# Weight splits and small set-up steps moved in the opening of a fused delta-rule attention, MLP and routed-expert kernel

## What is computed

```python
# 1: delta-rule attention, for each of the 32 batch*head pairs
k_n = k / (norm(k) + 1e-06)
for t in range(S):
    y[t] = q[t] @ state
    state += beta[t] * outer(k_n[t], v[t] - k_n[t] @ state)
# 2: MLP on the 3072 tokens (384 -> 2048 -> 384)
h = x @ w_in
x = maximum(0.01 * h, h) @ w_out
# 3: skip test, then the best of 8 experts (384 -> 1024 -> 384) for each token kept
do_compute = x @ w_skip > 0
e = argmax(xc @ w_gate); out = xc + gate_w * (relu(xc @ w1[e]) @ w2[e])
```

## Time and profile before

| | us |
|---|---|
| median of 3 runs | 889.0 |
| lowest and highest of the three | 887.79 and 889.74 |
| the profiled execution | 887.79 |
| its span, first to last instruction | 886.0 |

### The profile page before, as it was taken

One profiled execution on the slowest core, in us unless ns is written; L12 is line 12 of the kernel. 1 busy time (PEld: TensorE's weight loads), 2 busy tenths in 40 slices (PEclk: granted clock), 3 DMA queues, 4 the chain that ended last, 5 costly groups with the idle time before them and its releaser, 6 DMA issues.

```text
span 886.0 us, 27697 instructions
## 1 busy us (share of the span) xinstructions
PE 776.4 (88%) x10782; PEld 624.0 (70%) x10783; DVE 661.4 (75%) x1333; ACT 496.1 (56%) x1108; POOL 416.3 (47%) x498
## 2 busy tenths in 40 slices
PE   0134689999999999999999999999999899999985
PEld 0134567777878787777787788878777677778764
DVE  6758978888888888888888787866868773553382
ACT  4543566667676767666666666555465552442261
POOL 5212254545362636354554535352353665565473
PEclk9995799999999999999999999999999999999998
DMA  9869666676777697767677676336515864363100
GB/s 214 222 115 209 130 103 115 131 132 128 131 133 147 135 138 148 128 129 135 129 130 123 129 138 123 77 66 208 180 29 205 273 231 157 104 197 113 40 17 17
DMA packets 357245, 119.76 MB, mean 135 GB/s; under 512 B 330418, under 2 KB 348388, under 8 KB 356752
## 3 DMA queue, kind: packets, MB, share of 16 engines
q1 hardware_dynamic: 351424, 104.33, 56.6%
q0 software_dynamic: 3200, 7.64, 2.6%
q10 hardware_dynamic: 2512, 6.29, 2.1%
HBM read 63.53 MB, written 21.25 MB: 96 GB/s over the span
## 4 chain that ended last, share of the span: by engine, by line
PE 35%; DVE 23%; issue 11%; ACT 9%; DMA 9%; SPq 7%; POOL 5%; DVEq 0%; POOLq 0%; ACTq 0%
PE b_acc L848 8%; PE b_h L742 7%; PE b_acc L755 7%; PE b_h L835 6%; DVE stage L1484 4%; PE b_ch L681 4%; SPq L497 3%; DVE inv L1410 3%; DVE inv L1416 3%; DMA t_dram<-inv 3%; ACT ga L953 2%; ACT operands L953 2%; DMA operands<-t_dram 2%; ACT stage L1073 1%; PE b_gr L643 1%
## 5 line engine op out<-in xcount | busy, mean ns | idle before, releaser
L1908 POOL TENSOR_TENSOR stage<-stage 128x256 f16<-128x256 f32 x192 | 143.1, 746 | 251.2 <-ACT stage L953 250.3
L742 PE MATMUL b_h<-stage,wt 128*128 128x256 f16 x1728 | 222.3, 275 | 7.9 <-DVE stage L1343 5.4
L755 PE MATMUL b_acc<-wt,stage 128*128 128x384 f16 x1152 | 219.3, 327 | 2.5 <-POOL stage L1908 1.6
L742 PEld LDWEIGHTS b_h<-stage,wt 128*128 128x128 f16 x1728 | 159.1, 98 | 28.7 <-DVE stage L1343 7.5
L755 PEld LDWEIGHTS b_acc<-wt,stage 128*128 128x128 f16 x1152 | 107.0, 98 | 57.6 <-POOL stage L1908 4.5
L953 ACT ACTIVATE stage<-stage 128x256 f16<-128x256 f32 x192 | 80.0, 417 | 106.5 <-DVE stage L1484 105.5
L1484 DVE SCALAR_TENSOR_TENSOR stage<-b_h,stage 128x256 f32<-128x256 f32 x192 | 80.7, 420 | 42.1 <-ACT stage L1073 40.6
L848 PE MATMUL b_acc<-wt,operands 128*128 128x384 f16 x552 | 98.8, 330 | 7.3 <-DVE operands L1524 7.3
L835 PEld LDWEIGHTS b_h<-y,wt 128*128 128x128 f16 x1656 | 93.5, 98 | 6.5 <-issue 4.6
L835 PE MATMUL b_h<-y,wt 128*128 128x128 f16 x1656 | 96.5, 220 | 1.5 <-DVE y L1343 0.7
L1416 DVE TENSOR_REDUCE inv<-inv 128x30 f32<-128x90 f32 (+4 forms) x180 | 85.0, 472 | 5.8
(11 more groups left out here) (215 smaller groups left out, 1289.0 us busy)
## 6 DMA issues: line engine op xcount, KB each, us to landing
operands<-in_moe_w_dram SPq DMA_DIRECT2D x18, 1536.0 KB, 7.3
a_sys<-a_dram SPq DMA_DIRECT2D x24, 256.0 KB, 4.4
kc<-operands SPq DMA_DIRECT2D x22, 256.0 KB, 4.3
natq<-in_q_dram SPq DMA_DIRECT2D x24, 192.0 KB, 4.0
raw_v<-in_v_dram SPq DMA_DIRECT2D x24, 192.0 KB, 4.1
stage<-y SPq DMA_DIRECT2D x96, 48.0 KB, 2.0
x_dram<-stage SPq DMA_DIRECT2D x24, 192.0 KB, 2.9
out_dram<-stage SPq DMA_DIRECT2D x24, 192.0 KB, 3.4
```

The lines of the kernel that those rows point to most:

```text
L742: mm = pe.matmul(b_h[f % 2][:, 0:GT], wt[0][:, a, d * FF + f * P:d * FF + (f + 1) * P], xT[:, g % 2, b, d, :], start=(i == 0), stop=(i == ...
L755: mm = pe.matmul(b_acc[w][:, 0:DM], g16[:, f % 4, a, w * P:(w + 1) * P], wt[1][:, b, f * DM:(f + 1) * DM], start=(f == 0 and (a, b) == PAR ...
L1908: pool.tensor_tensor(g16[:, f % 4, LO, :], g32[:, f % 4, :], g16[:, f % 4, HI, :], ALU.subtract).then_inc(g_lo, 1)
```

## The change

Six things are moved or exchanged; the arithmetic is the same.

1. `split_w_in(2)` goes behind the start of W_out's load on ACT, and behind `norm(2)` on DVE.
2. `a21_high(0)` goes ahead of `q_high(0)` on ACT, and `a21_low(0)` from behind `inverse_low(0)` to a place ahead of `q_low(0)` and of the inverse on DVE.
3. `split_w_out(0)` and `(1)` on ACT go from ahead of `inverse_high(0)` to behind the last `p_high(0)`, with `seed(1)` between them. On DVE they stay where they were.
4. The zeroing of `kn[2]` goes from POOL to DVE.
5. In its place POOL issues a plain DMA of 128 single values (`row_id`, ready by then) to a new scratch tensor in DRAM that nobody reads. Its completion adds 16 to `yo_scattered`.
6. The waits on `yo_scattered` count 16 more, and tile 0, which had none, has one as well.

```diff
@@ ScalarE
             for st in range(B):
                 gram_out(0, st)
-            split_w_in(2)
+            a21_high(0)
             for x in range(2):
                 q_high(0, x)
             act.wait_ge(const_pool, 1)
             seed(0)
-            a21_high(0)
             act.wait_ge(a_loaded[0], 32)
             load_w_out(0)
+            split_w_in(2)
             squares(2)
             first_z()
-            for i in range(2):
-                split_w_out(i)
             inverse_high(0)
...
             for st in range(2, B):
                 p_high(0, st)
+            split_w_out(0)
             seed(1)
+            split_w_out(1)
             act.wait_ge(t_loaded, 128)
             load_w_out(1)
@@ VectorE
             kn_low(1)
             split_w_in(1)
-            split_w_in(2)
+            zeros(kn[2])
+            a21_low(0)
             for x in range(2):
                 q_low(0, x)
             inverse(0, 0, LINKS)
             inverse_low(0)
-            a21_low(0)
             for r in range(2):
                 scan_z_low(0, r)
             norm_sum(2)
             norm(2)
+            split_w_in(2)
@@ GpSimd
-            pool.memset(kn[2].bitcast(F32), 0.0).then_inc(zeroed, 1)
+            pool.dma_start(spare_dram, row_id[:]).then_inc(yo_scattered, 16)
...
-                if not (isinstance(t, int) and t == 0):
-                    pool.wait_ge(yo_scattered, 16 * t)
+                pool.wait_ge(yo_scattered, 16 * t + 16)
                 pool.sem_inc(yo_left, 1)
...
-            pool.wait_ge(yo_scattered, 16 * total)
+            pool.wait_ge(yo_scattered, 16 * total + 16)
```

More of the change, by code:

```diff
@@ L72, in build @@
         t_dram = nc.dram_tensor("t_dram", (2, 4, NU, 2, HR, BLK), F16, kind="Internal").ap()
+        spare_dram = nc.dram_tensor("spare_dram", (P, 1), F32, kind="Internal").ap()
         ident = sb("ident", [P, P])
```

## The result

| | before | changed |
|---|---|---|
| median of 7 runs each, us | 887.79 | 895.81 |
| lowest and highest, us | 886.92, 889.74 | 891.07, 896.93 |
| the profiled execution, us | 887.79 | 895.62 |
| its span, us | 886.0 | 893.9 |
| the same, to the start of the first W_in matmul | 98.06 | 105.50 |

The changed kernel takes 1.0075 times as long, 95% interval 1.0052 to 1.0097 (an estimate from all runs of both kernels; the two medians alone would give 1.0090). The forecast was 889.8, the range 887.2 to 892.2: the time lies above both. Of 7.9 us more of span, 7.44 are there when the first W_in matmul starts (98.06 before, 105.50 now), and the rest of the program took 788.4 against 787.9. So the loss is in the opening, as everything in the argument was. All lines of the changed kernel are one higher than before, POOL's behind the new DMA two.

What follows compares the result with a forecast made beforehand. DVE's in-order list up to the first W_in matmul was taken as the bound, SP's chain second. Terms +0.6 (with -1.37 in it), 0, 0, 0.2 and 0 gave +0.8 us: forecast 889.8, range 887.2 to 892.2.

Steps and rivals of the forecast that it cites:

- the small DMA's price: POOL's new DMA just before a_sys is read: delays a_sys by 0.2 us, bounds 0 and 0.92.
- Rival C: The extra DMA holds up a_sys, so the inverse starts after 37; 2.6 us in place of 0.2, 892.2 us; chance 0.12.
- What bounds the kernel: Opening up to the first W_in matmul: DVE's in-order list bounds, SP's chain 0.92 us behind; shifts carry unchanged to the end.
- Ahead of the inverse: DVE before the block inverse: 0.84 us more work fits in idle time; the inverse still starts when a_sys lands, cost 0.
- a21_low: Leaves the chain between inverse and norm_sum, so root, gram_out(1) and masked tiles come 1.37 us earlier; bounds 0 and 1.37.
- Rival D: The 1.37 us isn't gained, as POOL at nat_k(2) or PE's gram tiles end as late; 891.1 us; chance 0.11.
- split_w_in(2) behind norm(2): DVE's 2.29 us piece fits in 3.03 us of idleness, slowing nat_k(2) on POOL to 3.29; cost 0, other end 0.7.
- The two W_out copies: On ACT between last p_high and u's high half: +1.95 us before any gain, net +0.6 with the 1.37 counted in.
- Tile loop: One fused register step per tile in POOL's sequencer, 97 ns at most, 20 times; taken as 0, far end 0.6.

Runs made afterwards that it cites:

- h1: The changed kernel with the small DMA's 128 values of 4 bytes each written to a row of 512 bytes of its own; 889.70 us, ratio 1.0022.
- f2: The changed kernel with the same 128 values sent from ACT's queue, ahead of a21_high(0), instead of POOL's; 898.19 us, ratio 1.0112.
- h2: The changed kernel with only 8 of the small DMA's 128 values written, side by side; 891.08 us, ratio 1.0031.

## Why the prediction was wrong, step by step

**The failed step is the small DMA's price.** The sum had it at 0.2 us, from the cost of a packet on q1 and q0, bounds 0 and 0.92. It measured 6.67 at the inverse. The DMA's packets did cost next to nothing: the trace has 32 of them, two for each of 16 engines and not 8, and they were gone before 30 us. What cost was the word of completion, and no row of the queues' shares holds that. Rival C had the mechanism (the stores' landing holds up a_sys), but priced it by the landing of the scatter, 2.6 us. That scatter writes whole rows, so the row was of the wrong kind. And the argument against C, "8 short packets per engine", took short for cheap, where many short writes side by side are what is dear. The sign that it gave for C, an inverse that starts after 37, is the one that came. With 6.67 in place of 0.2 the sum gives 0.6 + 6.67, or 895.1 for the profiled execution, which took 895.62.

**What bounds the kernel: right.** The opening's shift reached the end nearly one for one: from the first W_in matmul to the end of the span it was 787.9 before, 788.4 in the changed kernel, 787.5 without the DMA, 789.6 with the DMA alone. Over all profiled executions it lies between 785.0 (h1) and 790.1 (f2, h2), so this holds for a shift of 7 us and can't be read from single executions for one under 2. And DVE's list with SP's chain close behind was confirmed by moving the W_out piece.

**Ahead of the inverse: right, 0.** Without the DMA it starts at 36.06 with all three moved pieces ahead of it.

**a21_low: the size was off.** 1.37 predicted. ACT's wait ahead of root fell from 4.04 to 2.62, so all of it arrived there. By the last masked tile 1.19 was left in the changed kernel, and in the kernel with a21 alone 0.92 counted from the start of the inverse (33.39 to 68.68 - 36.21 = 32.47), in the one without the DMA 0.82 (68.63 - 36.06 = 32.57). In those two PE took most of the rest: its second gram tile for the queries, in the kernel before and in the one without the DMA:

```profile
60.51 0.91 PE L643 MATMUL b_ch<-operands 128*128 128x128 f16 x12
```

```profile
59.24 1.47 PE L644 MATMUL b_ch<-operands 128*128 128x128 f16 x12
```

Twelve matmuls of the same shape take 0.56 us longer when they start 1.27 us earlier. The granted clock is 1.00 in both stretches, so it isn't the clock; what it is wasn't tried. Rival D had said that PE's gram tiles could end as late as before; it was half right.

**split_w_in(2) behind norm(2): right, 0.** nat_k(2) took 3.38 (3.3 predicted), ended at 66.57, and ACT came to it at 68.18. The rule in the Trainium skill (SBUF — State Buffer, Who interferes with whom) agrees with this row too: DVE's piece was issued at 63.01, POOL's at 63.19, and POOL waited for it.

**The two W_out copies: right.** +1.95 predicted ahead of any gain, 1.95 measured from the last masked tile to the second low half of u. (That low half stood at 74.98 before, where the sum had 75.06, so its +0.6 should have been +0.7.) The first piece waits for ACT (2.07 idle) and the low half of u for its high half (0.93, about 1 predicted). The collision with POOL is gone, as said: the pieces take 1.76 and 1.75 where they took 2.48 and 2.24, and POOL's two p_low 2.27.

**Tile loop: 0, not contradicted.** The rest of the program differs by 0.5 us, less than single executions scatter. Nor did the small DMA help the first gather on the same queue: its issue took 1.22 us at 647.57 before and 1.13 at 655.87 now.

So the five other terms add up to 0.77 at the first W_in matmul (1.95 - 1.19 + 0.01), against 0.6 predicted. In the kernel without the DMA they add up to 1.26: 0.12 at the start of the inverse, -0.82, 1.94 and 0.02 on the same stretches. There the gain from a21_low, which the sum had at 1.37, was worth 0.82.

## What to carry to other kernels

An extra DMA has to be priced by the completions that it delays, not by its bytes: ask which store stands behind it on the same 16 engines and who waits for that store's semaphore. Where a transfer has no other use than to exist, give it rows of 512 bytes, or put its small values 512 bytes apart, or read instead of write: at this place that is 0.1 to 0.5 us at the inverse instead of 6.7. When a wait ends late while the windows show a DMA share of 0.00, look at what was written just before, on any queue.

## What was unexpected of the hardware

- 128 values of 4 bytes written to one stretch of 512 bytes took 5.5 us to be acknowledged (30.40 to 35.87), 0.36 us apart in the mean, and held back stores issued on another queue until 38.05. The same values 512 bytes apart took 0.21 us (30.39 to 30.60).
- 8 of these values side by side take 0.14 us (30.07 to 30.21): eight writes don't show it, 128 do.
- The delay also reached transposes: 9.65 us for two that took 4.82, when the small DMA went ahead of them.
- The pace of PE's small gram matmuls (12 in 0.91 or 1.47 us at a granted clock of 1.00) isn't explained by the clock.
